# Starting the second network's first token pair before the last hidden step of the first network, and running its output products one pair later

## The reference

```python
# 1 decayed linear attention, for each head h with gamma_h
state = gamma * state + outer(k_t, v_t);  y_t = scale * q_t @ state
x = y, heads side by side                     # (3072 tokens, 512)
# 2 first network
h = x @ w_in                                  # (3072, 2048)
g = where(h >= 1, h, where(h <= -1, 0, (h + 1)**2 / 4))
x2 = g @ w_out                                # (3072, 512)
# 3 second network
h = x2 @ w2_in                                # (3072, 1024)
e = exp(h - max(h));  solu = h * e / (sum(e) + 1e-9)
ln = (solu - mean(solu)) / sqrt(var(solu) + 1e-6) * g_ln
out = ln @ w2_out                             # (3072, 512)
```

## Time and profile before

| | us |
|---|---|
| median of 3 runs | 887.69 (886.99, 887.69, 890.6) |
| the profiled execution | 891.81 |
| its span (what the rows cover) | 890.0 |
| TensorE busy in it | 864.4 |
| VectorE, ScalarE, GpSimd busy | 447.4, 333.1, 242.5 |

### The profile page before, as it was taken

One profiled execution on the slowest core, in us unless ns is written; L12 is line 12 of the kernel. 1 busy time (PEld: TensorE's weight loads), 2 busy tenths in 40 slices (PEclk: granted clock), 3 DMA queues, 4 the chain that ended last, 5 costly groups with the idle time before them and its releaser, 6 DMA issues.

```text
span 890.0 us, 12101 instructions
## 1 busy us (share of the span) xinstructions
PE 864.4 (97%) x4816; PEld 704.5 (79%) x4816; DVE 447.4 (50%) x772; ACT 333.1 (37%) x505; POOL 242.5 (27%) x234
## 2 busy tenths in 40 slices
PE   8999999999999999999999999998779999999988
PEld 7788878888888888888887888887568888888866
DVE  4545443334323343333433244656588888778751
ACT  2333342213221232122222132444456666666542
POOL 2644532222232223222212122248111111122000
PEclk9999999999999999999999999999979999999989
DMA  9921111111112102111111004310445544444442
GB/s 335 353 80 51 48 48 48 49 60 36 60 48 62 69 9 87 49 48 36 60 36 36 24 1 143 100 42 1 140 139 159 157 151 143 143 141 143 150 148 93
DMA packets 50744, 82.85 MB, mean 93 GB/s; under 512 B 5248, under 2 KB 23680, under 8 KB 50688
## 3 DMA queue, kind: packets, MB, share of 16 engines
q1 hardware_dynamic: 50688, 82.08, 28.3%
HBM read 56.90 MB, written 25.17 MB: 92 GB/s over the span
## 4 chain that ended last, share of the span: by engine, by line
PE 90%; DVE 3%; DMA 2%; POOL 2%; issue 1%; ACT 1%; SPq 0%; DVEq 0%; ACTq 0%; POOLq 0%
PE acc L401 30%; PE h L371 28%; PE o_ps L895 14%; PE p L842 10%; PE att L308 3%; PE att L319 2%; PE att L343 1%; PE att L333 1%; POOL w_out_lo L720 1%; DVE solu L1047 1%; DMA q<-in_q 1%; DVE h L993 1%; DMA x_raw<-x2T 1%; DVE zT_lo L1077 0%; ACT solu L941 0%
## 5 line engine op out<-in xcount | busy, mean ns | idle before, releaser
L401 PE MATMUL acc<-g_hi,w 128*128 128x512 f32 x768 | 257.2, 396 | 0.0
L371 PE MATMUL h<-x_hi,w 128*128 128x512 f32 x760 | 249.9, 389 | 0.5 <-DVE x_lo L581 0.5
L708 POOL TENSOR_TENSOR g_lo<-g_raw,g_hi 128x512 fp32r<-128x512 f32 x96 | 124.4, 1296 | 395.2 <-ACT g_hi L440 395.2
L497 ACT ACTIVATE g_raw<-g_raw,half_bias 128x512 f32<-128x512 f32 x96 | 69.6, 724 | 334.1 <-DVE g_raw L648 334.1
L401 PEld LDWEIGHTS acc<-g_hi,w 128*128 128x128 f32 x768 | 144.1, 188 | 35.1 <-issue 3.4
L371 PEld LDWEIGHTS h<-x_hi,w 128*128 128x128 f32 x760 | 142.6, 188 | 30.6 <-DVE x_lo L581 0.9
L648 DVE TENSOR_SCALAR g_raw<-h 128x512 f32<-128x512 f32 x96 | 66.2, 689 | 168.1 <-PE acc L401 167.9
L401 PE MATMUL acc<-g_lo,w 128*128 128x512 f32 x384 | 149.6, 390 | 0.0
L371 PE MATMUL h<-x_lo,w 128*128 128x512 f32 x380 | 147.9, 389 | 0.0
L653 DVE TENSOR_TENSOR g_raw<-h,g_raw 128x512 f32<-128x512 f32 x96 | 66.4, 692 | 70.0 <-ACT g_raw L497 70.0
L895 PE MATMUL o_ps<-w_out_hi,zT_hi 128*128 128x512 f32 x192 | 77.3, 403 | 15.7 <-DVE zT_lo L1077 11.9
(11 more groups left out here) (116 smaller groups left out, 1061.2 us busy)
## 6 DMA issues: line engine op xcount, KB each, us to landing
z<-zq SPq DMA_DIRECT2D x24, 512.0 KB, 3.5
zt<-z SPq DMA_DIRECT2D x96, 128.0 KB, 3.1
kT<-in_kT SPq DMA_DIRECT2D x24, 256.0 KB, 2.7
q<-in_q SPq DMA_DIRECT2D x24, 256.0 KB, 2.6
v<-in_v SPq DMA_DIRECT2D x24, 256.0 KB, 3.0
x2T<-y SPq DMA_DIRECT2D x24, 256.0 KB, 2.5
x_raw<-x2T SPq DMA_DIRECT2D x12, 512.0 KB, 3.8
out<-o SPq DMA_DIRECT2D x24, 256.0 KB, 2.1
```

Source lines behind the costliest of these rows:

```text
L371: last = mm(hb[f % 2][:, :], ww, xx[:, kt, :], start=kt == 0 and t == 0, stop=kt == KT - 1 and t == 2)
L401: last = mm(acc[m][:, :], ww, gg[:, f % 2, :], start=f == 0 and t == 0, stop=f == FT1 - 1 and t == 2)
L497: nc.scalar.activation(gate[:, f % 2, :], gate[:, f % 2, :], ACT.Square, bias=half_bias[:, 0:1], scale=0.5).then_inc(sem["squared"], 1)
L708: tt(g[1][:, f % 2, :], gate[:, f % 2, :], g[0][:, f % 2, :].bitcast(F32), ALU.subtract)\
```

## The change

- **Last step.** On every engine the sixth block's loop ends one step early (`steps(blk)`). The pieces of step 15 go to `finish` and are put into phase two's queues: on TensorE up(0) comes first, then up(5, 15), down(5, 13), down(5, 14), down(5, 15); on VectorE the clamp stands between the two `soften` of pair 0 and the `larger` behind `variance(0, SECOND)`; on ScalarE square and high part stand behind `squares(0, SECOND)`; on GpSimd the low part stands behind four pieces of `w2_out_lo` and one root.
- **Banks of pair 0.** Its seven products use three banks only: pb0, pb1, pb2, pb0, pb1, pb2, pb0, with waits on `gmax` of step 14, `part_copied` and `taken` between them.
- **A pair later.** TensorE's order becomes up(1), up(2), down(0), up(3), down(1), down(2), up(4), and so on to up(9), down(13), down(14), up(10), up(11), down(15) to down(23). There are five `zT` buffers, ScalarE's `output` and SyncE's `store` follow. `part` and `part7` are halves of `e`.
- **Preparation.** The output weights load one step earlier and are scaled two, three, three at steps 9, 10, 11 instead of two each at 10 to 13; x parts move one to two steps ahead; GpSimd's sums from steps 11, 13 to 10, 12.
- **SyncE.** `load_x2(2)` no longer waits for the end of phase one; the sixth block's `store_x2` stands behind `get_z(1)`.
- **Tail.** For the last pair ScalarE, VectorE and SyncE have an order of their own, in which outputs of tiles 15, 16, 17 stand between the pieces of pair 11.

```diff
             def dense(blk):
-                for f in range(FT1):
+                for f in range(steps(blk)):
...
-            finish["down"] = lambda: [down(BLOCKS - 1, f) for f in range(FT1 - LAG, FT1)]
+
+            def last_step():
+                up(BLOCKS - 1, FT1 - 1)
+                for f in range(FT1 - LAG - 1, FT1):
+                    down(BLOCKS - 1, f)
+
+            finish["pe_last_step"] = last_step
...
-                if 11 <= f < 15:
-                    for piece in (2 * (f - 11), 2 * (f - 11) + 1):
-                        act.wait_ge(sem["w2_scaled"], piece + 1)
-                        copy(mem["w2_out"][0][:, piece, :], mem["w2_out_raw"][:, piece, :])\
-                            .then_inc(sem["w2_out_hi"], 1)
-                if f in (13, 15):
-                    n = (f - 13) // 2
+                for piece in {10: (0,), 12: (1, 2, 3), 13: (4,), 14: (5, 6, 7)}.get(f, ()):
+                    act.wait_ge(sem["w2_scaled"], piece + 1)
+                    copy(mem["w2_out"][0][:, piece, :], mem["w2_out_raw"][:, piece, :])\
+                        .then_inc(sem["w2_out_hi"], 1)
+                if f in (11, 13):
+                    n = (f - 11) // 2
...
-                if f == 10:
+                if f == 9:
                     dve.wait_ge(sem["gains"], 16)
-                if 10 <= f < 14:
-                    for piece in (2 * (f - 10), 2 * (f - 10) + 1):
+                for piece in {9: (0, 1), 10: (2, 3, 4), 11: (5, 6, 7)}.get(f, ()):
...
-                if f >= 14:
-                    n = f - 14
+                if f in (12, 14):
+                    n = (f - 12) // 2
...
-                        for piece in {12: (0, 1), 14: (2, 3), 15: (4, 5)}.get(f, ()):
-                            finish["pool_w2_out"](piece)
-                        if f in (11, 13):
-                            finish["pool_sums"]((f - 11) // 2)
+                        if f in (10, 12):
+                            sums_of_x2((f - 10) // 2)
+                        for piece in {13: (0, 1), 14: (2, 3)}.get(f, ()):
+                            w2_out_lo(piece)
...
+        def bank_of(n, product):
+
+            return pb[((0, 1, 0, 1, 2, 2, 0) if n == 0 else (0, 1, 1, 4, 5, 2, 3))[product - 1]]
...
                 if n == 0:
-                    pe.wait_ge(sem["gmax"], BLOCKS * FT1)
-                product(pb[2], s(1), t(1))
-                product(pb[3], s(2), b(0, RIGHT))
+                    pe.wait_ge(sem["gmax"], BLOCKS * FT1 - 1)
+                product(bank_of(n, 6), s(1), t(1))
                 if n == 0:
                     pe.wait_ge(sem["part_copied"], 1)
                 if n == 1:
+                    pe.wait_ge(sem["gmax"], BLOCKS * FT1)
+                product(bank_of(n, 7), s(2), b(0, RIGHT))
+                if n == 0:
+                    pe.wait_ge(sem["taken"], 1)
+                if n == 1:
                     for par in range(2):
                         pe.wait_ge(sem["acc_free"][par], 2 * BLOCKS)
-                product(bank4(n), a(1, SECOND), t(2))
-                pe.wait_ge(sem["taken"], 5 * n + 1)
-                product(bank5(n), s(0), t(0))
+                product(bank_of(n, 4), a(1, SECOND), t(2))
                 if n == 0:
                     pe.wait_ge(sem["taken"], 2)
-                product(bank3(n), s(3), b(1, RIGHT))
+                product(bank_of(n, 5), s(0), t(0))
+                pe.wait_ge(sem["taken"], 5 * n + (1 if n else 3))
+                product(bank_of(n, 3), s(3), b(1, RIGHT))
...
-            for n in range(PAIRS2 - 1):
+            for n in range(PAIRS2):
                 up(n)
                 if n == 0:
-                    finish["down"]()
-                if n >= 2:
-                    down(2 * n - 3)
-                if 1 <= n < PAIRS2 - 2:
-                    down(2 * n - 2)
-            up(PAIRS2 - 1)
-            for s in range(TILES - 6, TILES):
+                    finish["pe_last_step"]()
+                if 3 <= n < PAIRS2 - 2:
+                    down(2 * n - 5)
+                if 2 <= n < PAIRS2 - 2:
+                    down(2 * n - 4)
+            for s in range(TILES - 9, TILES):
                 down(s)
...
+            join(0)
+            soften(0, SECOND)
+            finish["dve_clamp"]()
+            soften(0, FIRST)
+            variance(0, SECOND)
+            finish["dve_larger"]()
```

More of the change, by code:

```diff
@@ L24 @@
 LAG = 2
-LAG2 = 3
+Z_TILES = 5
 SQ = 32
@@ L487, in prepare, with square, high @@
                         .then_inc(sem["x2_hi"], 1)
+            def square(blk, f):
+                wait(act, sem["clamped"], blk * FT1 + f + 1)
+                nc.scalar.activation(gate[:, f % 2, :], gate[:, f % 2, :], ACT.Square,
+                                     bias=half_bias[:, 0:1], scale=0.5).then_inc(sem["squared"], 1)
+            def high(blk, f):
+                wait(act, sem["gmax"], blk * FT1 + f + 1)
+                copy(g[0][:, f % 2, :], gate[:, f % 2, :]).then_inc(sem["g_hi"], 1)
             def dense(blk):
-                for f in range(FT1):
-                    n = blk * FT1 + f
+                for f in range(steps(blk)):
                     if f == FT1 - 1 and blk < BLOCKS - 1:
@@ L495, in dense @@
                         evacuate(blk - 1)
[L496 to L500, removed]
+                    square(blk, f)
+                    high(blk, f)
                     if blk == 0:
@@ L634, in prepare, with clamp, larger @@
                        mem[f"x2_sum{n}"][0][:, :, :, :].bitcast(F32), ALU.subtract).then_inc(sem["x2_lo"], 1)
+            def clamp(blk, f):
+                n = blk * FT1 + f
+                wait(dve, sem["h_ready"], n + 1)
+                wait(dve, sem["g_used"], n - 1)
+                nc.vector.tensor_scalar(gate[:, f % 2, :], hb[f % 2][:, :], 1.0, -1.0, ALU.min, ALU.max)\
+                    .then_inc(sem["clamped"], 1)
+            def larger(blk, f):
+                wait(dve, sem["squared"], blk * FT1 + f + 1)
+                tt(gate[:, f % 2, :], hb[f % 2][:, :], gate[:, f % 2, :], ALU.max).then_inc(sem["gmax"], 1)
             def dense(blk):
-                for f in range(FT1):
-                    n = blk * FT1 + f
-                    h = hb[f % 2][:, :]
+                for f in range(steps(blk)):
                     if f == FT1 - 1 and blk < BLOCKS - 1:
@@ L645, in dense @@
                         evacuate(blk - 1)
[L646 to L649, removed]
+                    clamp(blk, f)
                     if blk < BLOCKS - 1:
                         attention(blk + 1, 2 * f + 1)
-                    wait(dve, sem["squared"], n + 1)
-                    tt(gate[:, f % 2, :], h, gate[:, f % 2, :], ALU.max).then_inc(sem["gmax"], 1)
+                    larger(blk, f)
                     if blk == 0 and f + W_READY < FT1:
@@ L700, in split_weights, with low @@
                     .then_inc(sem["w_out_lo"], 1)
+            def low(blk, f):
+                wait(pool, sem["g_hi"], blk * FT1 + f + 1)
+                tt(g[1][:, f % 2, :], gate[:, f % 2, :], g[0][:, f % 2, :].bitcast(F32), ALU.subtract)\
+                    .then_inc(sem["g_lo"], 1)
             def dense(blk):
-                for f in range(FT1):
+                for f in range(steps(blk)):
                     if blk < BLOCKS - 1:
@@ L706, in dense @@
                         attention(blk + 1, 2 * f + 1)
-                    wait(pool, sem["g_hi"], blk * FT1 + f + 1)
-                    tt(g[1][:, f % 2, :], gate[:, f % 2, :], g[0][:, f % 2, :].bitcast(F32), ALU.subtract)\
-                        .then_inc(sem["g_lo"], 1)
+                    low(blk, f)
                     if blk == 0:
```

205 lines of the change are left out of this document (131 added, 74 removed).

## The result

| | us |
|---|---|
| kernel before, median of 19 runs | 888.38 (885.88 to 891.42) |
| changed kernel, median of 19 runs | 885.97 (884.39 to 888.14) |
| ratio | 0.9975, 95% interval 0.9965 to 0.9986 |
| profiled execution of the changed kernel | 886.03, span 884.2, TensorE busy 862.4 |

The change saves 2.4 us, by the interval 1.2 to 3.1. The forecast was 1.4 us less, 886.3. It is faster than before by less than 0.5%, inside the range and in the class that the forecast held likeliest.

What follows compares the result with a forecast made beforehand. TensorE, busy 97% of the span, bounds the kernel; only its idle and lower-clock time can be won. New stalls of 25.9 us against 27.3 wasted give 1.4 less, 886.3 from the median 887.69; range 883.5 to 889.5.

Steps and rivals of the forecast that it cites:

- A: up(5,13) waits because preparation brought forward delays step 11's clamp: stall of 2.2 us, plus 1.7 for the clock.
- B: up(0) on three banks: P4 waits 1.1 us for P1's copy, P5 0.2 to 0.3; 1.4 in all, no clock loss.
- C: Last step: down(5,15) waits for g's low part, covered only by down(5,14): stall of 2.95 us, clock 2.3.
- D: up(2) directly behind up(1): P7 waits for the join to read its bank; 4.55 us, P2 about 0.1, clock 2.8; 7.4.
- E: up(11) directly behind up(10): P7 waits for the join to read its bank; 4.55 us, P2 about 0.1, clock 2.8; 7.4.
- F: P7 of up(3) waits because VectorE runs late behind D: 0 to 2.6 us, taken as 0.5.
- Removed: All seam and tail stalls of the kernel before go, among them 11.9 us for z and 3.7 for an output copy.
- Rival 1: Milder stalls: A 0.6 with clock kept, B 1.3, other gaps lose 1.7 each, F 0; 879.6 us; chance 0.18.
- Rival 4: The change does all its order says, with no new waits: 860.4 us; chance 0.03.
- rival 2: One of D and E does not arise, VectorE's pair being through sooner: saves 7.4, 879 us; both 871.5; chance 0.08.
- Rival 3: The clock doesn't recover in up(0), making it slower; chance 0.13, two thirds of it beyond 892 us.

Runs made afterwards that it cites:

- experiments 10 and 11: Kernel before and changed kernel each run once more, unaltered: 888.45 us and 884.96 us.
- experiment 2: Changed kernel with output products half a pair later instead of a whole one, output and store in step: 874.85 us, ratio 0.9844 to the kernel before.
- experiment 1: Changed kernel with down(15) put back between up(10) and up(11) on TensorE: 879.03 us, ratio 0.9902 to the kernel before.
- experiment 4: Changed kernel with VectorE's output-weight scalings spread two, one, three, two over steps 9, 10, 11, 13: 884.27 us in one execution.
- experiment 5: Changed kernel with GpSimd's four sums of x2_0 moved from step 10 to step 11: 886.69 us in one execution.
- experiments 8 and 9: Changed kernel with step 15 ahead of up(0) again, 885.91 us; the same with the sixth block's accumulator copies moved forward, 885.07 us.
- experiment 7: Changed kernel with output products half a pair later, soften before clamp, scalings spread; ScalarE's last three weight pieces moved behind the copy of P1: 871.44 us.
- experiment 3: Changed kernel with soften(0, FIRST) ahead of step 15's clamp on VectorE: 883.8 us in one execution.

## Why the prediction was right, and where it was not

The forecast was 1.4 us less; measured are 2.4, with 1.2 to 3.1 as interval. The mechanism came out as forecast: which waits go, which come, where, and on what. The number is near in part by luck, as shown below. The terms in us, idle as the waits show it; the second profile of each kernel is that of experiments 10 and 11:

| part | forecast idle | measured idle, two profiles | forecast clock | lost, two profiles |
|---|---|---|---|---|
| A, up(5,13) | 2.2 | 1.90, 1.90 | 1.7 | 0, 0 |
| B, up(0) | 1.4 | 1.05, 1.03 | 0 | 0, 0 |
| C, down(5,15) | 2.95 | 2.58, 2.57 | 2.3 | 1.7, 1.6 |
| D, P7 of up(2) | 4.65 | 4.22, 4.21 | 2.8 | 1.7, 1.7 |
| E, P7 of up(11) | 4.65 | 4.20, 4.20 | 2.8 | 1.6, 1.4 |
| F, P7 of up(3) | 0.5 | 1.20, 1.32 | 0 | 0, 0 |
| sum | 16.35 | 15.15, 15.23 | 9.6 | 5.0, 4.7 |

The forecast counts a stall from the time at which the matmul was due, the idle column from the modelled end of the matmul in front, which is 0.16 later (0.39 long for a successor at 0.227): the idle terms agree to 0.3 us each but for F. (Of the 1128 matmuls left at 603.67, 48 are of phase one and not 36; the total, on which the 27.3 us rest, is right.)

- **Removed.** Right: the waits for z and for the output are gone, z is nearly ready behind up(1) already (experiment 2), and nothing took their place in the tail (experiment 1).
- **A.** Right in place and size; experiments 4 and 5 show its cause. The working behind the size is right only in sum. It lets GpSimd's sums slow the low part ahead of the scalings from 1.47 to 2.32 us, and the three scalings to 2.0. In the changed kernel the low part took 1.47 as before, and the scalings 2.71: 0.85 too much and 0.7 too little. (The diff moves these sums from step 11 to step 10, not from 12.) Wrong in the clock: this gap lost nothing in both profiles. In experiments 8 and 9 the same gap lost 1.7. The low part in the changed kernel:

```profile
587.95 1.47 DVE L640 TENSOR_TENSOR w_sum_lo<-w_sum_raw,w_sum_hi 128x1024 fp32r<-128x1024 f32 x1 [1.65 <-ACT w_sum_hi L458]
```

- **B.** Right in P4's wait; P5, for which the forecast added 0.2 to 0.3, did not wait behind it. That the first addition is the bound next to it, experiment 7 shows.
- **C.** Right in the chain (experiment 3); its clock was priced at 2.3 for 1.7 and 1.6.
- **D and E.** Right in mechanism and idle time (experiments 1 and 2). The clock's loss was taken from the one gap of 3.72 and was 1.1 to 1.4 too large in these profiles.
- **F** was mis-sized, 0.5 for 1.2 to 1.3. It hangs on D's clock: VectorE fixes when the next join can start, so what the clock loses less behind D, TensorE waits more at up(3). The sum stays:

| kernel | lost behind D | F idle | sum |
|---|---|---|---|
| changed, two profiles | 1.7, 1.7 | 1.20, 1.32 | 2.9, 3.0 |
| experiment 1 | 2.5 | 0.56 | 3.1 |
| experiment 3 | 3.0 | none | 3.0 |
| experiment 4 | 2.5 | 0.64 | 3.1 |
| experiment 5 | 1.7 | 1.41 | 3.1 |

The forecast had 3.3 for both together, so this mistake cost little.

The term that failed in size is the clock's. The forecast read it off one execution of the kernel before, at 891.81 slower than all 19 that were timed, in which all three large gaps had lost, and priced D and E close to the largest of these losses and A and C by them too. For the new gaps that is 9.6 where the profiles lost 5.0 and 4.7; for the old ones it is 7.3, where the second profile lost 5.6. In the forecast the clock takes 2.3 back of the gain in idle time; by the two pairs of profiles it adds 2.3 and 0.9 to it.

**Where luck comes in.** The forecast took a difference that it had sized on the slow execution, 27.3 of waste, off a median that lies 4.1 lower. By the table the changed kernel wastes about 5 us less than the forecast had: 15.15 and 5.0 for 16.35 and 9.6, with 0.16 more for each gap by the way of counting. With that right, the same subtraction would have given 6 us less, which is the 5.8 between the two profiled executions and not the 2.4 between the medians. The new waste was overrated and so was that of an ordinary execution before, and the two mistakes nearly cancel.

**The clock of the timed executions.** The record has the granted clock of each, averaged over the span. For the changed kernel the mean of 19 is 0.9924, where both its profiles have 0.994; for the kernel before it is 0.9896 in the 52 executions that were timed beside the experiments, where its profiles have 0.985 and 0.988. So the average execution of the changed kernel loses more at the lower clock than its profiles, by about 1.3 us, and that of the kernel before less than either of its own. This is the direction that is wanted: idle time alone is 18.7 less 15.2, 3.5 us, the two pairs of profiled executions differ by 5.8 and 3.5 us, and the medians of 19 by 2.4. So on the average the clock seems to take back a part of the gain, as the forecast said. How much is lost behind which gap stays open, since these means also hold idle time and the start of the span.

**The rivals.** Rival 1 (879.6) did not come as a time, but its clock terms are those of both profiles: nothing behind A, about 1.7 behind each of C, D and E. Its A and F were too small (0.6 and 0 for 1.9 and 1.2), and it too was taken off the median. Rival 4 (860.4) did not come, and of rival 2, D and E were both whole; its 879 is what experiment 1 measured (879.03) where E was taken away. Rival 3 did not come either: behind B's gap of 1.05 the granted clock stayed at 1.00 in all eight profiles that have it.

The Trainium skill, in TensorE: Matmul & The Clock Gate, section on PSUM-queue depth-cycling, tells of a kernel that cycled through banks in each iteration, with frequent short idle times between groups of matmuls, and whose clock swung. up(0) cycles three banks with one such gap, and its clock did not fall; many gaps in a row, as the Trainium skill has them, no run here shows.

What the GPSIMD Engine Reference of the Trainium skill says in its Specifications, that GpSimd contends in SBUF with VectorE's instructions in a two-port mode or with two SBUF inputs, agrees with experiment 5 as far as it goes: three scalings took 2.71 us beside GpSimd's sums and 1.26 without. In which mode they ran no trace shows.

## What to carry to other kernels

Before consumers are delayed to hide a long transfer, ask what they stood between: an output product between two pairs was also the time in which VectorE freed a bank, and moving it away turned a stall of 0.3 us into two of 4.2. Delay by as much as the transfer needs and no more: in this kernel half a pair measured 11 us less than a whole one. And take idle gaps from a trace, but the clock's loss behind them only as a range from several executions; and take a difference off the time of the same execution on which its terms were read, or read both sides on several.

## What the runs showed of the hardware that was not expected

- Most of TensorE's gaps that hang on other engines' queues repeat within 0.03 us in the two profiles of a kernel (F and the waits for the output and for z within 0.12 to 0.17); the clock's loss behind them does not. In single profiles gaps up to 1.72 us lost nothing; gaps from 1.89 to 2.89 lost 0 or 1.7, and both happened at one and the same gap (C, 2.58, and the 2.2 before the change); gaps of 3.9 to 4.2 lost 1.4 to 3.1, those of 3.6 to 12.1 before the change 2.6 to 3.0.
- Which of the two pays for working side by side differs. The first of GpSimd's four sums, 0.74 us in the earlier trace rows, took 1.72 beside VectorE's low part and the first scaling in the changed kernel, and that low part kept its 1.47; beside the later sums VectorE's scalings paid (2.71 for 1.26):

```profile
588.30 1.72 POOL L761 TENSOR_TENSOR x_sum_raw<-x_raw 128x256 f32<-128x256 f32 x1
589.98 0.92 POOL L763 TENSOR_TENSOR x_sum_raw<-x_raw 128x256 f32<-128x256 f32 x1
```
